# Dilated-attention and adapter kernel: two scratch products fewer at the start, and five loads in six runs per partition

## What is computed

```
scores = scale * q @ k.T                       # (8, 8, 576, 576)
mask_plain = (rel >= 0) & (rel < 32)           # heads 0 to 3
mask_dil = (rel >= 0) & (rel < 128) & (rel % 4 == 0)   # heads 4 to 7
attn = softmax(where(mask, scores, -1e9));  x = attn @ v    # x: (4608, 512)
logits = x @ w_gate;  topk = the two largest of 8;  w = softmax of the two
out = x + sum over the two of  w * ((x @ A[e]) @ B[e])      # rank 16 each
```

## Time and profile before

| | before |
|---|---|
| median of three runs | 100.47 us (100.41 to 103.09) |
| profiled execution, first to last instruction | 99.2 us |
| TensorE busy | 81.6 us (82%) |
| ScalarE, VectorE, GpSimd busy | 71.0, 62.3, 54.6 us |
| HBM read, written | 29.07 MB, 9.44 MB |
| DMA packets | 5807, 24.50 MB |

### The profile page before, as it was taken

One profiled execution on the slowest core, in us unless ns is written; L12 is line 12 of the kernel. 1 busy time (PEld: TensorE's weight loads), 2 busy tenths in 40 slices (PEclk: granted clock), 3 DMA queues, 4 the chain that ended last, 5 costly groups with the idle time before them and its releaser, 6 DMA issues.

```text
span 99.2 us, 3611 instructions
## 1 busy us (share of the span) xinstructions
PE 81.6 (82%) x1587; PEld 59.9 (60%) x1587; DVE 62.3 (63%) x138; ACT 71.0 (72%) x123; POOL 54.6 (55%) x73
## 2 busy tenths in 40 slices
PE   3999969959569989999897979999799989766200
PEld 2443457548356765779676859878687878545100
DVE  5770007706468189359746697779676999979700
ACT  5195494399938983896997679989689899757200
POOL 5999900880549136404942297099085574637800
PEclk9999999999999999999999999999999999999975
DMA  2999999999999999999999999999979988979991
GB/s 33 300 204 208 207 214 226 201 217 220 211 211 211 214 219 213 219 216 206 210 217 212 224 212 214 210 204 175 198 264 412 415 353 360 426 297 401 420 422 76
DMA packets 5807, 24.50 MB, mean 247 GB/s; under 512 B 800, under 2 KB 928, under 8 KB 5024
## 3 DMA queue, kind: packets, MB, share of 16 engines
q0 software_dynamic: 3920, 14.23, 71.9%
q1 hardware_dynamic: 1728, 9.77, 23.9%
q10 hardware_dynamic: 144, 0.28, 1.0%
HBM read 29.07 MB, written 9.44 MB: 388 GB/s over the span
## 4 chain that ended last, share of the span: by engine, by line
PE 57%; ACT 18%; DVE 9%; DMA 5%; issue 3%; POOL 2%; POOLq 0%
PE ps L213 49%; ACT p L351 11%; PE ps L414 5%; DMA out_dram<-x 5%; DVE x L551 4%; DVE x L390 3%; ACT xt L424 2%; PE ps L504 1%; ACT zs L472 1%; POOL x L559 1%; ACT in L263 1%; POOL xb L397 1%; PE ps L438 1%; ACT xt L427 1%; DVE top L492 1%
## 5 line engine op out<-in xcount | busy, mean ns | idle before, releaser
L397 POOL CAST xb<-x 128x1152 bf16<-128x1152 f32 (+1 forms) x16 | 18.3, 1144 | 25.4 <-DVE x L390 25.4
L351 ACT ACTIVATE p<-ps 128x960 bf16<-128x960 f32 (+1 forms) x32 | 27.6, 899 | 4.2 <-PE ps L213 4.1
L213 PE MATMUL ps<-in,p 128*64 128x130 bf16 (+1 forms) x416 | 21.5, 221 | 3.7 <-ACT p L351 3.1
L390 DVE TENSOR_TENSOR x<-ps,rec 128x1152 f32<-128x1152 f32 x16 | 21.7, 1358 | 0.5
L213 PEld LDWEIGHTS ps<-in,p 128*64 128x64 bf16 (+1 forms) x416 | 17.1, 104 | 7.2 <-ACT p L351 4.1
L551 DVE TENSOR_TENSOR x<-x,ps 128x1024 f32<-128x1024 f32 (+1 forms) x16 | 17.5, 1116 | 3.4 <-PE ps L213 3.4
L387 DVE RECIPROCAL rec<-ps 128x18 f32<-128x18 f32 x16 | 4.3, 270 | 17.5 <-PE ps L213 17.3
L213 PE MATMUL ps<-warm 128*128 128x512 f32 x22 | 13.1, 737 | 1.5 <-DVE warm L217 1.5
L499 POOL TENSOR_TENSOR gz<-zs,g 128x640 bf16<-128x640 f32 x7 | 8.9, 1275 | 9.4 <-DVE g L494 9.4
L213 PEld LDWEIGHTS ps<-in 64*64 64x64 bf16 x576 | 10.9, 106 | 2.9 <-issue 0.9
L213 PE MATMUL ps<-in 64*64 64x96 bf16 (+1 forms) x576 | 11.9, 201 | 0.7 <-issue 0.7
(11 more groups left out here) (55 smaller groups left out, 101.8 us busy)
## 6 DMA issues: line engine op xcount, KB each, us to landing
out_dram<-x SPq DMA_DIRECT2D x6, 1152.0 KB, 6.1
in<-in_qkv_dram POOLq DMA_DIRECT2D x5, 1152.0 KB, 22.1
in<-in_qkv_dram POOLq DMA_DIRECT2D x10, 292.5 KB, 23.1
in<-in_qkv_dram POOLq DMA_DIRECT2D x10, 288.0 KB, 8.2
out_dram<-x SPq DMA_DIRECT2D x4, 576.0 KB, 3.8
in<-in_qkv_dram POOLq DMA_DIRECT2D x10, 146.2 KB, 8.1
in<-in_qkv_dram POOLq DMA_DIRECT2D x2, 434.2 KB, 13.7
awf<-in_aw_dram ACTq DMA_DIRECT2D x1, 272.0 KB, 3.8
```

Source lines behind the costliest of these rows:

```text
L213: return nc.tensor.matmul(o, lhsT=lhsT, rhs=rhs, start=start, stop=stop, skip_group_check=True)
L351: return [nc.scalar.activation(p[:, :, :].rearrange("p h (s c) -> p h s c", c=PER)[:, :, b0 : b0 + nb, 0:SEG], PS[:, k.at : k.at + 2, 0 : ...
L390: nm = add(f"N{tag}", "DVE", ("el", XG), lambda: [nc.vector.tensor_tensor(X[r][:, XG * g : XG * g + XG].rearrange("p (b i n) -> p b i n", ...
L397: add(f"B{tag}", "POOL", ("el", cut), lambda: [nc.gpsimd.tensor_copy(XB[r % 2][:, g, 0:cut], X[r][:, XG * g : XG * g + cut])], [nm] + free)
```

## The change

FILL loses its first entry, which was F1 with two products; the others keep their places in PLAN under new numbers (F2 becomes F1, F3 becomes F2). The host puts gaps in the middle of each q/k piece and of the v piece of rows 2 to 6, and the loads of these rows name the halves one by one: four runs of 1152 elements for q and k in place of two of 2304, and two of 1170 for v in place of one of 2340. Destination, order and number of the loads stay.

```diff
-FILL = (("S000", 2), ("V01", 2), ("S111", 1), ("S130", 1))
+FILL = (2, 1, 1)
...
-    for i, (_, n) in enumerate(FILL):
+    for i, n in enumerate(FILL):
...
-                out=IN[r % SLOTS][:, 2 * VB : 2 * VB + 2 * QK].rearrange("p (j n) -> p j n", j=2),
-                in_=qkv[r].rearrange("a p n -> (a p) n")[:, 0 : 2 * (QK + PAD)].rearrange("p (j n) -> p j n", j=2)[:, :, 0:QK],
+                out=IN[r % SLOTS][:, 2 * VB : 2 * VB + 2 * QK].rearrange("p (j n) -> p j n", j=4),
+                in_=qkv[r].rearrange("a p n -> (a p) n")[:, 0 : 4 * (HQK + PAD)].rearrange("p (j n) -> p j n", j=4)[:, :, 0:HQK],
...
-                out=IN[r % SLOTS][half(h), ROW * h : ROW * h + 2 * VB],
-                in_=qkv[r, h, :, 2 * (QK + PAD) : 2 * (QK + PAD) + 2 * VB],
+                out=IN[r % SLOTS][half(h), ROW * h : ROW * h + 2 * VB].rearrange("p (j n) -> p j n", j=2),
+                in_=qkv[r, h, :, 4 * (HQK + PAD) : 4 * (HQK + PAD) + 2 * (VB + PAD)].rearrange("p (j n) -> p j n", j=2)[:, :, 0:VB],
...
-pz0 wz warm@4 F1@1 awf btf vz00 pz2 con vz10 Lk00 Lk01 Lv00 Lv01
+pz0 wz warm@4 awf btf vz00 pz2 con vz10 Lk00 Lk01 Lv00 Lv01
...
-F2@1 L10 cd1 S100@4 S101@6 E100 E101 L2 Lw2 S001@2 E001 V00@4 R00 N00 V01@1
+F1@1 L10 cd1 S100@4 S101@6 E100 E101 L2 Lw2 S001@2 E001 V00@4 R00 N00 V01@1
```

More of the change, by code:

```diff
@@ L25 @@
 QK = 4 * S
+HQK = 2 * S
 VB = 2 * NB * VW
@@ L611 @@
 Y01 m01 Y11 m11 L5 Lw5 s121 S020@1 D02@0 V21@5 E120 top1 tt1 th1 g21
-E020 A02 V20@0 R21 N21 R20 gz1 G1@5 gn1 F3@6 S130@6 N20 gc1 B21 E130
+E020 A02 V20@0 R21 N21 R20 gz1 G1@5 gn1 F2@6 S130@6 N20 gc1 B21 E130
 S031@3 D12@2 E031 S030@0 D10@5 T21@7 E030 C21 A12 S131@3 B20 V30@0 A10 E131
@@ L660, in layout @@
     a = np.stack([np.concatenate(low, -1), np.concatenate(high, -1)], 1)
-    whole = np.zeros((B, 2, 64, ROW + 3 * PAD), a.dtype)
+    whole = np.zeros((B, 2, 64, ROW + 6 * PAD), a.dtype)
     whole[..., :ROW] = a
@@ L666, in layout @@
                 x = QK_AT[h][g] - 2 * VB * h
-                whole[r, h, :, g * (QK + PAD) :][:, :QK] = a[r, h, :, x : x + QK]
-            whole[r, h, :, 2 * (QK + PAD) :][:, : 2 * VB] = a[r, h, :, y : y + 2 * VB]
+                for i in range(2):
+                    whole[r, h, :, (2 * g + i) * (HQK + PAD) :][:, :HQK] = a[r, h, :, x + HQK * i : x + HQK * i + HQK]
+            for i in range(2):
+                whole[r, h, :, 4 * (HQK + PAD) + i * (VB + PAD) :][:, :VB] = a[r, h, :, y + VB * i : y + VB * i + VB]
     return whole
```

## The result

| | before | after |
|---|---|---|
| median of the runs, taken in turns on one chip | 100.9 us (100.16 to 103.34) | 101.24 us (100.31 to 102.5) |
| ratio, 95% interval | | 1.0046 (1.0028 to 1.0064) |
| profiled execution, first to last instruction | 99.2 us | 99.4 us |

The change makes the kernel 0.5% slower, where 0.5% faster was forecast. It is inside the forecast's "within 2%", but its sign is the other one, and the interval excludes no change.

The account below looks back on a forecast made before the run. Loads then stores fill the DMA engines end to end, with compute close beside them. A lead of 0.6 us less 0.1 for GpSimd, with the stream's +0.3 not adding, gave 100.47 - 0.5 = 100.0 us; range 99.2 to 101.3.

Parts of the forecast that it names:

- within 2%: Whole kernel: the measured time differs from the kernel before by no more than 2%, about 2 us; chance 0.93.
- The step that failed: Row 2 onward: no load holds compute, so the 0.6 us lead, less 0.1 for GpSimd, stays 0.5.
- the stream or the fetches get smoother: Rival, TensorE's stalls and the load stream: half-length packets shorten instruction-fetch stalls, stream 1.2 us faster; time 99.2; chance 0.2.
- The start: Rows 0 and 1: scratch removal saves 1.7 us, row 1's data takes part back, compute 0.6 us ahead at row 2.
- E010: Step on ScalarE at 24.15 behind a copy: forecast to follow S010 directly at about 23.2, up to 0.9 us earlier.
- GpSimd: Load issues of rows 2 to 6: 0.42 us longer a row, mostly hidden, 0.1 us charged to compute behind L6.
- The stream: Loads of rows 2 to 6: 120 more packets per DMA engine make the stream 0.3 us later.
- The end: Last stores: first stores 0.2 us earlier, A53 and O3 both at 87.3, O5 issued at 87.35 in place of 87.9.
- The base: Starting time: a median of 100.47 us, 1.3 over the profiled span of 99.2, from which 0.5 was taken.
- The short packets cost more: Rival, load stream: decides once the stream loses over 0.8 us; 101.1 at 1.5 us, 101.9 at 2.3; chance 0.17.
- the clock did not fall: Rival, TensorE between 11 and 23 us: longer waits drop its clock, compute +1.5 us, time 101.5; chance 0.05.
- The change does nothing: Rival, row 1 and GpSimd: waits of S111 and S010 and longer issues take the 0.5 us back; 100.5; chance 0.08.

Follow-up runs that it names:

- the short products with three runs: The kernel before, with the two scratch products ahead of S000 kept but cut to 16 columns in place of 512: ratio 1.0002 (0.9966 to 1.0037).
- the twenty small ones: The kernel before, with 20 small bf16 matmuls (64 rows, 96 columns) in place of the two scratch products ahead of S000: ratio 1.002 (0.998 to 1.006).
- the two-run kernel: The kernel before, with q/k of rows 2 to 6 in one run per partition in place of two, v as before: ratio 1.0008 (0.9963 to 1.0053).

## Why the prediction was wrong

- **The step that failed** is "From row 2 on the loads come some us ahead of need, and I find no other load that would hold compute." It let a lead of 0.5 us at row 2 stand until O5. What arrives late is no load of data but TensorE's own code, and it holds compute at records 855, 982 and 1235, for 2.4 us in all. Of 0.73 us nothing reaches O5, which leaves 0.35 later than before.
- **The same stall was read with the wrong sign.** The rival "the stream or the fetches get smoother" named the 0.55 us of the earlier trace rows as a possible fetch, and priced it as a gain of up to 0.8 us from shorter packets. The fetch was right; it is a bound on compute. The length of the load packets has no clear effect on it: the three pieces start 3.0 to 3.6 us after the border before with three runs, 3.0 to 3.9 with six.
- **The start** was right: 1.7 us of scratch, S000 forecast at 8.6 and found at 8.87, S111 and S010 behind their landings (forecast not before 18.4 and 22.5, found 18.31 and 22.50), E010 forecast at 23.2 and found at 23.23. The lead was forecast at 0.6 less 0.1, and is 0.73.
- **GpSimd** was charged 0.42 us a row and 0.1 us to compute; it took 0.2 us a row, and nothing of compute is seen to wait for it.
- **The stream** was charged 0.3 us. Row 7's loads land 0.3 to 0.5 later, and the runs alone cost 0.47 us by the timed ratio. The rule of the Trainium skill named in the prediction (DMA: Bandwidth & Descriptors, Why small descriptors are slow: three cycles a packet, 0.4 us as an estimate by that page) agrees with 3 to 4 ns a packet here. The size was right, but with the lead gone there was nothing to pay it with. One reading under it was off: the stream was thinnest before the third q/k load of row 7 landed (185 GB/s from 66 to 69 us, 194 from 69 to 71), so its 0.5 us do not all lie between that landing and the fourth; and 2.8% of 42 us is 1.2.
- **The end.** A53 still releases O5, as forecast, and O3 has landed 0.6 before. But O5 was forecast at 87.35 and left at 88.2: 0.5 of the miss is the lead that was lost, 0.35 the longer third stall. "So the end moves with O5" holds only roughly: with O5 0.35 later the profile ends 0.14 later, and with O5 0.98 and 1.03 later (the short products with three runs, the twenty small ones) 0.2 and 0.3 later, as the part of the stores that lags before and after does not lag there.
- **The base.** 100.47 was the median of three runs; over the 22 taken in turns the same kernel has 100.9. And the 1.3 us between its span and that median is not the time outside the span: every execution on record is 1.7 to 1.9 longer than its span. The forecast ratio, 0.995, does not hang on this; 0.43 of the 1.24 us between 100.0 and 101.24 does.
- **The rivals.** "The short packets cost more" had the sign right and a time near the measured one, 101.1, but by luck: it decided only from 0.8 us of stream loss on, since it kept the lead, and there were 0.3 to 0.5. After the change the clock did not fall: 1.00 from 7.4 to 96 us, although TensorE waited for data before S111 and S010. "The change does nothing" was closest in time, with its gain eaten at another place than the one it named.

What stays open: by which path six runs cost their 0.47 us in the run that has them alone; whether the two products' removal costs anything by itself; what holds a piece of code back in a dense stream for 3 to 4 us while its packet takes 1; why a part of the last store lags in some executions and what the 0.35 us of compute are worth with it; and what a kernel would do with the lead if no border stood in a dense stream. No kernel tried here beats the one before with the full work.

## What to carry to other kernels

Where a chain of waits shows stalls that nothing in the profile releases, count the engine's instructions between them: an equal number points to code that is being fetched, and then the borders, not the data, set the pace, and a lead won ahead of one is lost at it. Before counting a gain at the start, name every supply that runs on its own time up to the end (data, code, stores), and look for the place where each is last. On the full stream of this kernel each further packet cost 3 to 4 ns on its DMA engine, so splitting runs needs a reason that pays for it.

## What was not expected of the hardware

- TensorE's code came in pieces of 16 KB, about 127 pairs of weight load and matmul, over the same DMA engines as the data. Under 210 GB/s of loads TensorE needed 5.2 to 6.5 us from border to border where it had to wait, in the two kernels compared, and up to 7.4 in others; with 84 GB/s the stalls were gone, and a piece started as early as 0.7 us after a border.
- A border cost 0 to 2.05 us; in the two kernels where one stalled at 80 to 83 us, in the last steps of the work, it cost 1.6 and 1.97 us. Kernels that differed only in small products at the start were 0.2% to 5.3% slower.
- The clock fell behind two stalls for code: 1.72 us at 62 us was followed by a granted clock of 0.67 in the mean of 66 to 70 us, and 1.70 us at 51.8 in the profile of the two-run kernel by 0.69 from 52 to 56. The stall of 2.05 us in the run with twenty small products was not (1.00 from 66 to 78 us), so the stall's length alone doesn't decide.
- S000's own start varies between executions by 1.3 us with the same code (9.16 to 10.42 with the products, 8.08 to 8.87 without), with the moment from which the scratch's weight loads take 0.19 us in place of 0.34 (after 4.8 us where S000 stands at 9.16, after 6.8 where it stands at 10.42): the two levels of TensorE's clock. Nothing of this variation was seen to reach the end of the kernel.
- The last store landed 3.4 us after its issue in eight profiles and 3.9 to 5.2 in nine, with one of its 16 completion packets 0.5 to 1.4 us behind the others. In two kernels without the lag compute ended 1.0 us later than before, and the spans were only 0.2 and 0.3 us longer.
